# Stacked tail and a router with its matrix stationary, in an attention, mixture and gating kernel

## The reference

```
scores = q @ k.T / 8                       # 4 x 8 heads, 576 x 576, head size 64
scores below max - tau are masked; softmax; attn @ v      -> x [4, 576, 512]

logits = x @ w_gate                        # 512 x 8
local_gate = sigmoid(x @ w_local)          # 512 x 1
# per row: the argmax expert, or the previous row's if local_gate >= 0.5
out = p[e] * (relu(x @ w1[e]) @ w2[e])     # 8 experts, 512 x 1024 x 512

h = gelu(x @ w_in)                         # 512 x 1024
u, v = halves of h                         # 512 columns each
v_n = (v - mean) / sqrt(var + 1e-6) * g_ln
v_s = w_sg @ v_n + b_sg                    # 576 x 576, over the rows of a batch
y = x + (u * v_s) @ w_out
```

## Time and profile before

| | us |
|---|---|
| median of 3 runs | 932.36 |
| lowest, highest | 927.72, 933.27 |
| profiled execution | 926.78 |
| its span | 925.0 |
| TensorE busy | 903.1 |
| VectorE, ScalarE, GpSimd busy | 557.8, 413.2, 382.1 |

### The profile page before, as it was taken

One profiled execution on the slowest core, in us unless ns is written; L12 is line 12 of the kernel. 1 busy time (PEld: TensorE's weight loads), 2 busy tenths in 40 slices (PEclk: granted clock), 3 DMA queues, 4 the chain that ended last, 5 costly groups with the idle time before them and its releaser, 6 DMA issues.

```text
span 925.0 us, 16395 instructions
## 1 busy us (share of the span) xinstructions
PE 903.1 (98%) x6080; PEld 769.0 (83%) x6080; DVE 557.8 (60%) x1205; ACT 413.2 (45%) x788; POOL 382.1 (41%) x347
## 2 busy tenths in 40 slices
PE   8999999999999989999999999999999999999998
PEld 7889988898888877888888888788869888798796
DVE  6988788868868647536654789450035445445253
ACT  5877677767757632343334433333323132132130
POOL 5553357735643224455565565454204013040000
PEclk9999999999989999999999999999999999999999
DMA  7243223332340055526644566430040030210101
GB/s 177 59 104 91 66 66 80 114 99 64 83 116 15 14 174 185 189 73 194 221 143 143 172 225 201 132 104 19 1 115 2 1 103 1 64 40 1 52 1 52
DMA packets 47757, 86.82 MB, mean 94 GB/s; under 512 B 8124, under 2 KB 16444, under 8 KB 47680
## 3 DMA queue, kind: packets, MB, share of 16 engines
q1 hardware_dynamic: 43520, 76.02, 28.1%
q0 software_dynamic: 4000, 9.45, 3.2%
q10 hardware_dynamic: 160, 0.30, 0.1%
HBM read 73.42 MB, written 15.99 MB: 97 GB/s over the span
## 4 chain that ended last, share of the span: by engine, by line
PE 58%; DVE 3%; DMA 2%; issue 1%; ACT 0%; DVEq 0%; POOLq 0%
PE ps_y L1479 4%; PE ps_y L1481 4%; PE ps_y L1480 4%; PE ps_h L1440 4%; PE ps_h L1442 4%; PE ps_h L1441 4%; PE ps_a L1759 4%; PE ps_a L1761 4%; PE ps_a L1760 4%; PE ps_v L1759 4%; PE ps_v L1760 2%; PE ps_v L1761 2%; PE ps_r L1759 2%; PE ps_ht L1424 2%; PE ps_r L1760 2%; PE ps_r L1761 2%
## 5 line engine op out<-in xcount | busy, mean ns | idle before, releaser
L556 ACT COPY probs_t<-ps_ring 128x512 f32<-128x512 f32 x192 | 104.8, 562 | 69.8 <-PE ps_ring L652 64.3
L855 DVE TENSOR_REDUCE max_tau<-ps_s 128x1 f32<-128x576 f32 x144 | 108.3, 752 | 31.6 <-PE ps_s L605 31.0
L1365 DVE CAST w_high<-w_raw 128x1024 fp32r<-128x1024 f32 (+1 forms) x63 | 64.1, 1032 | 90.5 <-PE ps_h L1442 43.8
L869 DVE SCALAR_TENSOR_TENSOR probs<-ps_s,floor,expd 128x576 f32<-128x576 f32 x144 | 116.7, 810 | 1.7 <-ACT expd L507 1.4
L507 ACT ACTIVATE expd<-ps_s,max_tau 128x576 f32<-128x576 f32 x144 | 107.9, 749 | 8.9 <-DVE max_tau L855 8.5
L604 PE MATMUL ps_s<-k_high,q_split 128*128 128x288 f32 x336 | 105.7, 333 | 1.8 <-DVE q_split L810 0.9
L683 PE MATMUL ps_ring<-probs_t,v_pair 128*64 128x144 f32 x1280 | 93.8, 294 | 0.0
L605 PE MATMUL ps_s<-k_low,q_split 128*128 128x288 f32 x336 | 91.8, 296 | 0.0
L1632 POOL TENSOR_TENSOR rstd<-var_eps,exponent 128x1 f32<-128x1 f32 (+1 forms) x20 | 17.0, 849 | 171.9 <-DVE var_eps L1696 171.9
L1373 DVE TENSOR_TENSOR w_low<-w_raw,w_high 128x1024 fp32r<-128x1024 f32 x66 | 86.0, 1324 | 3.2 <-issue 3.2
L683 PEld LDWEIGHTS ps_ring<-probs_t,v_pair 128*64 128x64 f32 x1280 | 76.5, 138 | 10.6 <-issue 8.1
(11 more groups left out here) (273 smaller groups left out, 2106.3 us busy)
## 6 DMA issues: line engine op xcount, KB each, us to landing
w_raw<-in_w SPq DMA_DIRECT2D x63, 512.0 KB
k_in<-in_k SPq DMA_DIRECT2D x28, 288.0 KB, 4.2
q_in<-in_q SPq DMA_DIRECT2D x28, 288.0 KB, 4.3
v_pair<-in_v SPq DMA_DIRECT2D x16, 256.0 KB, 2.8
x_rows_dram<-scratch SPq DMA_DIRECT2D x4, 1024.0 KB, 4.7
scratch<-in_dense SPq DMA_DIRECT2D x8, 384.0 KB
scratch<-y_rows_dram SPq DMA_DIRECT2D x3, 1024.0 KB, 5.9
out<-scratch SPq DMA_DIRECT2D x3, 1024.0 KB, 4.4
```

Of the source, the lines that this page charges most:

```text
L556: nc.scalar.copy(out, src).then_inc(evacuated, 1)
L855: nc.vector.tensor_reduce(max_tau[:, n % 4, 0:1], scores(n), AX_XY, ALU.max, negate=True).then_inc(maxed, 1)
L869: nc.vector.scalar_tensor_tensor(out=row_of(pair, w).rearrange("p (a c) -> p a c", a=2), in0=scores(n), scalar=floor[:, n % 4:n % 4 + 1], ...
```

## The change

Two things are joined.

First, the tail of the gating layer. The tail's 64 rows are copied twice side by side when the turned rows are written (`turned_tile`, `y_tile`), so that the input product gives v's tail on all 128 partitions, the same rows twice. GELU, statistics, scaling and the high part run over 128 partitions. The low part is then written over the lower half of the high part, on the partitions 64 to 127. The host writes the tail of w_sg twice as well. One matmul with 128 rows of contraction gives high high + low high, and a second with w_sg's low part adds the rest: two matmuls in place of three. (It adds low low too, which was left out.) The buffer `spatial` moves into the scratch area.

Second, the router. `w_route` is padded to 32 columns and is now the stationary side; chunk c works in column group c of the array, with 288 columns of x_t moving (item `part`, two a batch). The four partial results lie on four quarters of the partitions; ScalarE copies them to `parts`, and the item `logits` adds them up by a product with `lanes_sum`, four identity blocks on top of each other, loaded by one more DMA. The steps: parts at 15 and 17, logits at 24, the rows items at 22, 33, 40, 42 and 44. For the last batch: parts at 4 and 5 and `early` at 7.

```diff
-LOGITS_AT, ROWS_AT = (15, 17), (22, 24, 33, 42, 44)
+PART_AT, LOGITS_AT, ROWS_AT = (15, 17), 24, (22, 33, 40, 42, 44)
+LANES = P // DC
-LAST_EARLY_AT, LAST_SUM_AT, LAST_LOGITS_AT = (4, 6), 10, (12, 13)
+LAST_PART_AT, LAST_EARLY_AT, LAST_SUM_AT, LAST_LOGITS_AT = (4, 5), 7, 10, (12, 13)
...
+        sp.dma_start(lanes_sum[:], io["lanes_sum"]).then_inc(const_loaded, 16)
...
+            elif kind == "part":
+                out, src = parts[:, HALF * i:HALF * i + HALF], bank[:, 0:HALF]
+            elif kind in ("logits", "early"):
+                nc.scalar.copy(logits[0:TAIL, FULL, :], bank[0:TAIL, FULL * (E + 1):QT * (E + 1)])
+                out, src = logits[:, 0:FULL, :], bank[:, 0:FULL * (E + 1)].rearrange("p (t e) -> p t e", t=FULL)
...
-            elif kind == "logits":
+            elif kind == "part":
+                chunks = DC if of < B - 1 else DC - 1
                 if i == 0:
-                    pe.wait_ge(dve_took, taken_from_ring("pv", PIECES - 1, PAIRS * of + PAIRS - 1))
-                for t in LOGIT_TILES[i]:
+                    pe.wait_ge(dve_took, taken_from_ring("pv", PIECES - 1, PAIRS * of + chunks - 1))
+                src = x_t[of % 2]
+                for c in range(chunks):
+                    last = nc.tensor.matmul(bank[LANES * c:LANES * c + LANES, 0:HALF], w_route[:, c, :], src[:, c, HALF * i:HALF * i + HALF],
+                                            start=True, stop=True)
+            elif kind in ("logits", "early"):
+                lanes = P if kind == "logits" else P - LANES
+                pe.wait_ge(evacuated, out_of_ring("part", 1, of))
+                for t in range(QT):
                     r = rows(t)
-                    for c in range(DC):
-                        last = nc.tensor.matmul(bank[0:r, (E + 1) * t:(E + 1) * (t + 1)], x_t[of % 2][:, c, P * t:P * t + r], w_route[:, c, :],
-                                                start=(c == 0), stop=(c == DC - 1))
+                    last = nc.tensor.matmul(bank[0:r, (E + 1) * t:(E + 1) * (t + 1)], parts[0:lanes, P * t:P * t + r], lanes_sum[0:lanes, :],
+                                            start=True, stop=True)
...
-                pe.wait_ge(const_loaded, 32)
+                pe.wait_ge(const_loaded, 48)
...
+    def turned_tile(b, t):
+        bank = y_bank(b, t)[:, 0:DC * rows(t)]
+        if t < FULL:
+            return bank.rearrange("p (c q) -> p c q", q=P)
+        return bank.rearrange("p (c q) -> p c q", q=TAIL).unsqueeze(2).to_broadcast([P, DC, 2, TAIL])
+    def y_tile(part, t):
+        cols = y_t[part][:, :, P * t:P * t + P]
+        return cols if t < FULL else cols.rearrange("p c (h q) -> p c h q", h=2)
...
-            nc.vector.tensor_tensor(v_parts[1][0:r, t, :], v[0:r, t, :], v_parts[0][0:r, t, :].bitcast(F32), ALU.subtract).then_inc(v_split, 1)
+            low = v_parts[1][:, t, :] if t < FULL else v_parts[0][TAIL:P, t, :]
+            at = slice(0, P) if t < FULL else slice(TAIL, P)
+            nc.vector.tensor_tensor(low, v[at, t, :], v_parts[0][at, t, :].bitcast(F32), ALU.subtract).then_inc(v_split, 1)
...
-                    last = product(ps_a[0:r, (t + 1) % 2, 0:G], lambda p: y_t[p][:, c, P * t:P * t + r],
+                    last = product(ps_a[:, (t + 1) % 2, 0:G], lambda p: y_t[p][:, c, P * t:P * t + P],
...
-                        last = product(ps_v[:, half, 0:HALF], lambda p: v_parts[p][0:r, t, P * c:P * c + P],
-                                       lambda p: w_sg[p][0:r, t, HALF * half:HALF * half + HALF], t == 0, t == QT - 1)
+                        if t < FULL:
+                            product(ps_v[:, half, 0:HALF], lambda p: v_parts[p][:, t, P * c:P * c + P],
+                                    lambda p: w_sg[p][:, t, HALF * half:HALF * half + HALF], t == 0, False)
+                        else:
+                            for part in range(2):
+                                last = nc.tensor.matmul(ps_v[:, half, 0:HALF], v_parts[0][:, FULL, P * c:P * c + P],
+                                                        w_sg[part][:, FULL, HALF * half:HALF * half + HALF], start=False, stop=(part == 1))
...
+            if tile.shape[0] < P:
+                dense[TAIL:P, at:at + tile.shape[1]] = tile
...
-        "w_route": np.concatenate([moe_w_gate, moe_w_local], axis=1), "w1": moe_w1, "w2": moe_w2,
+        "w_route": np.concatenate([moe_w_gate, moe_w_local, np.zeros((D, P // DC - E - 1), np.float32)], axis=1),
+        "lanes_sum": np.tile(np.eye(P // DC, E + 1, dtype=np.float32), (DC, 1)),
```

More of the change, by code:

```diff
@@ L103, in step_items @@
         for i in range(2):
-            per_step[after_batch(b, LOGITS_AT[i])].append(("logits", i, b))
+            per_step[after_batch(b, PART_AT[i])].append(("part", i, b))
+        per_step[after_batch(b, LOGITS_AT)].append(("logits", 0, b))
         for i in range(QT):
@@ L114, in step_items @@
     for i in range(2):
-        per_step[after_batch(last, LAST_EARLY_AT[i])].append(("early", i, last))
+        per_step[after_batch(last, LAST_PART_AT[i])].append(("part", i, last))
+    per_step[after_batch(last, LAST_EARLY_AT)].append(("early", 0, last))
     per_step[after_batch(last, LAST_SUM_AT)].append(("ids", 0, last - 1))
@@ L218, in attention @@
     tau = sb("tau", [P, 1])
-    w_route = sb("w_route", [P, DC, E + 1])
+    w_route = sb("w_route", [P, DC, LANES])
+    lanes_sum = sb("lanes_sum", [P, E + 1])
     logits = sb("logits", [P, QT, E + 1])
@@ L275, in attention @@
     probs_t = [large(f"probs_t{i}", [P, W + 1, S]) for i in range(2)]
+    parts = large("parts", [P, S])
     pick_p, pick_c = large("pick_p", [P, QT, P], F32R), large("pick_c", [P, QT, COLS], F32R)
@@ L700, in fill @@
             elif kind == "late":
                 pe.wait_ge(dve_took, taken_from_ring("pv", PIECES - 2 + i, ALL_PAIRS - 1))
-                for t in LOGIT_TILES[i]:
+                for t in LATE_TILES[i]:
                     r = rows(t)
-                    last = nc.tensor.matmul(bank[0:r, (E + 1) * t:(E + 1) * (t + 1)], last_x[:, DC - 1, P * t:P * t + r], w_route[:, DC - 1, :],
+                    last = nc.tensor.matmul(bank[0:r, (E + 1) * t:(E + 1) * (t + 1)], last_x[:, DC - 1, P * t:P * t + r], w_route[:, DC - 1, 0:E + 1],
@@ L911, in argmax @@
             if b < B - 1:
-                dve.wait_ge(evacuated, out_of_ring("logits", 1, b))
+                dve.wait_ge(evacuated, out_of_ring("logits", 0, b))
             else:
@@ L1523, in gmlp @@
     y = [route["scratch"][:, QT * D * i:QT * D * (i + 1)].rearrange("p (t d) -> p t d", t=QT) for i in range(2)]
-    y_t = [sb(f"y_t_{part}", [P, DC, S], F32R) for part in ("high", "low")]
+    y_t = [sb(f"y_t_{part}", [P, DC, QT * P], F32R) for part in ("high", "low")]
     v = sb("v", [P, QT, G])
@@ L1528, in gmlp @@
     gated_parts = [sb(f"gated_{part}", [P, DC, S], F32R) for part in ("high", "low")]
-    spatial = sb("spatial", [P, 2, HALF])
+    spatial = route["scratch"][:, 2 * QT * D + S:2 * QT * D + 2 * S].rearrange("p (h s) -> p h s", h=2)
     stats = sb("stats", [P, QT, 6])
@@ L1629, in body @@
             for t in range(QT):
-                r = rows(t)
                 pool.wait_ge(eps_done, QT * b + t + 1)
-                nc.gpsimd.tensor_tensor(rstd[0:r, t:t + 1], var_eps[0:r, t:t + 1], exponent[0:r], ALU.pow).then_inc(rstd_done, 1)
+                nc.gpsimd.tensor_tensor(rstd[:, t:t + 1], var_eps[:, t:t + 1], exponent[:], ALU.pow).then_inc(rstd_done, 1)
         batches(pool, body)
@@ L1639, in y_high @@
             for t in tiles:
-                r = rows(t)
                 act.wait_ge(y_done, QT * b + t + 1)
-                nc.scalar.copy(y_t[0][:, :, P * t:P * t + r], y_bank(b, t)[:, 0:DC * r].rearrange("p (c q) -> p c q", q=r)).then_inc(y_high_done, 1)
+                nc.scalar.copy(y_tile(0, t), turned_tile(b, t)).then_inc(y_high_done, 1)
         nc.scalar.activation(warm[:], prob[0:1, 0:1], ACT.Gelu_apprx_tanh)
@@ L1651, in body @@
                 if n < QT:
-                    r = rows(n)
-                    nc.scalar.activation(v[0:r, n, :], bank[0:r, 0:G], ACT.Gelu_apprx_tanh).then_inc(a_out, 1)
+                    nc.scalar.activation(v[:, n, :], bank[:, 0:G], ACT.Gelu_apprx_tanh).then_inc(a_out, 1)
                     if b == 0 and n + 2 < QT:
@@ L1661, in body @@
                     if 0 <= t < QT:
-                        r = rows(t)
                         act.wait_ge(norm_done, QT * b + t + 1)
-                        nc.scalar.copy(v_parts[0][0:r, t, :], v[0:r, t, :]).then_inc(v_high_done, 1)
+                        nc.scalar.copy(v_parts[0][:, t, :], v[:, t, :]).then_inc(v_high_done, 1)
             for i in range(V_ITEMS):
```

39 lines of the change are left out of this document (8 added, 31 removed).

## The result

| | before | after |
|---|---|---|
| median of the timed executions, us | 932.13 | 905.33 |
| profiled execution | 926.78 | 905.45 |
| its span | 925.0 | 903.6 |
| TensorE busy | 903.1 | 878.1 |

One of the four timed executions of the changed kernel took 1725.84 us, with no trace that would show why; it is left out of the ratio, and the other three lie between 904.78 and 905.45. The ratio of the times is 0.9728 (95% interval 0.9702 to 0.9755; it is not the plain quotient of the two medians). The forecast was 908 in a range of 899 to 919. A later repetition, six executions against eleven of the kernel before, gave 904.13 against 931.11, ratio 0.9726 (0.9687 to 0.9765).

A forecast was written before the change was run, and what follows sets the result against it. TensorE's own instruction sequence was taken as the bound (busy 98%). Terms summed to -22.2 us, giving 904.6 from the profiled 926.8 or 910.2 from the median 932.4; forecast 908 us, range 899 to 919.

The forecast's parts named there:

- Stacked tail: Spatial product: 14 products of one height instead of 15 with switches, 0.52 us less in each of 32 groups, -16.5.
- The cover of the tail's low part: Spatial product: VectorE's low-part subtraction ends 2.7 us before TensorE asks for the tail, so no late start.
- v's tail, 128 wide: First product's tail: stationary of 64 columns becomes 128 wide; entering it costs no more than full ones, nothing to gain, 0.
- Router: Router logits in attention: parts at 0.82 us, summing product 1.18, 2.82 a batch instead of 4.20; -4.1 for three batches.
- Row items: Attention: row item moved from step 24 to 40 waits for ScalarE, +0.9 for two batches; third batch's leaves main stretch, -0.4.
- Start: First transposes: TensorE's wait for the router's matrix also covers one more small load, +0.6, ends 0 and +2.
- The ending: Attention's ending: two parts, a summing product and the row item replace 30 short entries, even, 0 (between -1 and +1).
- The clock: Third batch's router: half clock after the 24 nine-column entries goes, -2.7, with 0 as the other end.

The follow-up runs named there:

- both experiments: Changed kernel with three full-height tail matmuls: spatial stage 15.91 us; kernel before with two of three 64-row tail products: 17.84 us.
- the kernels with one, two and four groups: Changed kernel (four column groups) and it with a part's chunks adding up in one or two: step with a part 3.22, 2.26 and 1.78 us.
- the kernel with two narrow products: Kernel before with two of the tail's three 64-row products, w_sg's low part left out for the tail: spatial stage 17.84 us.
- the start experiment: Changed kernel with the first transposes waiting for the identity matrix only: 906.49 us.
- the tail alone: Kernel before with only the stacked tail and doubled w_sg rows, old router kept: 912.22 us against 931.11, ratio 0.9803.
- router alone: Kernel before with only the new router's hunks, tail as it was: 920.66 us, ratio 0.9898.
- The kernel with the nine columns back: Changed kernel with twelve old nine-column products put back ahead of the first part in each of the first three batches: 913.24 us.

## Why the prediction was right, step by step

**Stacked tail, forecast -16.5.** 4 x 4.06 = 16.2 in the stage and 0.11 a batch on leaving it for the row product, 16.7. The split into switch (0.39 a group, measured 3.00 / 8 = 0.375 within the stage) and matmul (0.13) held in both experiments. The cover of the tail's low part was enough: TensorE is busy for 14.85 of the stage's 14.85 us.

**v's tail, 128 wide, forecast 0.** The first batch's v and u products after their entry, 686.32 to 704.64 before, take 18.32, and 18.29 after. So the narrow fp32r stationary was not drained for. The Trainium skill, TensorEngine Tiling (Array Packing), section Key Properties, says that a change of the tiling mode drains the engine. That agrees with what the height costs here, 0.375 to 0.39 us a group; for this width of an fp32r stationary no run shows such a drain, and here the measurement decides.

**Router, forecast -4.1.** The steps give 3.66 + 2.52 - 2 x 1.78 - (2.17 - 0.99) = 1.44 a batch, -4.3. A part costs 0.79 where 0.82 was forecast, the summing product 1.18 as forecast. That four groups run side by side, which the prediction carried over from two, is shown by the kernels with one, two and four groups. The Trainium skill, TensorEngine Tiling (Array Packing), section Available Configurations, names four tiles of 128 x 32, and these runs agree: 0.69 us with four groups, 2.13 with one.

**Row items, forecast +0.9 and -0.4.** The step with `rest` and a row item takes 2.50, as in the earlier trace rows (120.23 to 122.73), 0.88 more than `rest` alone (1.62), while at a plain step the row item adds 0.43 (1.42 against 0.99). That is 0.45 more, as forecast.

**Start, forecast +0.6: the wait grew by 0.77 (1.59 to 2.36), but between these two profiles the path did not.** Here the step failed. The step before the first part begins at 102.94 before and 102.95 after. Half clock early in the attention (16.3 to 19.7 before, none after) blurs this a little. Without it the old wait gives 102.98 (the kernel with two narrow products) and the new one 102.83 to 103.00; with one such stretch the old wait gives 102.80 and 102.94, the new one 103.16 to 103.43. So of the 0.77 nothing came through in the first case, and some 0.2 to 0.6 in the second. I had read the wait as being on the path because TensorE stood still; behind it stood a wait for VectorE's masks, which the start experiment laid bare.

**The ending, forecast 0:** -0.2 (309.81 to 333.89 before, 302.19 to 326.10 after).

**The clock, forecast -2.7:** -3.1 in the two profiles, the step with the router's item included. A gain of 0.7 that was not forecast stands beside it: in the step at 172.5 a wait of 0.84 for VectorE, which the profile after has not.

Together -7.8 in the attention. The rest, +3.2, lies where the change does nothing: +1.8 in the experts (their scatter) and +1.4 at the entry of the gating layer, where the profile after has half clock from 670.1 to 673.5 and this one of before had none. The sum is -21.3, against the -22.2 of the forecast. Part of that agreement is luck: what the change touches gave -24.5, and the +3.2 elsewhere, which nobody forecast, took most of the difference back.

By the medians the gain is 26.8 and 27.0. The prediction's sum gave 904.6 on its profile and 910.2 on its median; the forecast of 908 took about half of the 5.6 us between them for half clock that would go, and 905.3 came out, near the lower end. Profile and median do not differ alike in all kernels (the tail alone was profiled 4.8 above its median, the repetition 3.3 below), but every timed execution has its granted clock on record. With the clock at 1.0 or 0.5, the time at half clock is 2 x (1 - granted clock) x span. The means over the executions:

| kernel | executions | granted clock | at half clock, us |
|---|---|---|---|
| before | 11 | 0.989 | 20.8 |
| tail alone | 7 | 0.990 | 18.8 |
| router alone | 6 | 0.994 | 10.4 |
| changed, repetition | 6 | 0.996 | 7.5 |

So it is the router's part that takes half clock away, some 10 to 13 us of it, and the tail's part next to none. In the third batch of before, 6.8 us of half clock cost 3.1 us. At that rate the 13.3 us between the first and the last row are worth about 6 us, an estimate. With the 16.7 and the 4.7 (the attention's 7.8 without its clock) that comes to 27. The clock term of the sum, 2.7, was thus what one profile showed and about half of what the average execution loses; the half of the offset that the forecast added made up for it. The traces tie the stretches in the attention to the router's products, by 7 of 12 against 0 of 24; that the executions without a trace have their extra half clock at the same place is argued, not shown. The kernel with the nine columns back, run once, has a granted clock of 0.994, no lower than the router alone.

## What to carry to other kernels

Read a matmul's cost as the distance to the next start, and look for the places where the distances are not those of the columns. A short tile in the contraction of an otherwise full product cost about as much by the two switches around it (0.375 us) as by its own three matmuls (0.39); stacking high and low parts made it a full one. A float32 product with nine moving columns was better turned around, its small side stationary and its chunks in separate column groups: 2.76 us a batch in place of 4.20. Before a wait is called part of the path, look for the next one behind it. Before a profile is set against a median, compare their granted clocks.

## What the runs showed of the hardware

- Going from 128 to 64 rows of contraction and back costs 0.375 to 0.39 us, and a 64-column fp32r stationary next to a 128-column one at most some 0.03 us (18.32 against 18.29 for the products that hold it).
- Four column groups of 32 run side by side on plain float32: eight entries of 288 columns in 0.69 us with four groups, 1.17 with two, 2.13 with one.
- Half clock came within 1.3 us of the end of a run of 24 nine-column entries in 7 of 12 cases, for 3.4 or 6.8 us, and near the parts in none of 24. TensorE was busy by the profile all through these stretches.
- The expert stage scatters by 4 us between executions of the same instructions, with between no and four waits for weights.
